# Token mixing of a Fourier layer: seven block products in place of eight, with the running results kept in DRAM

## The chip, the cores and the metric

The kernel runs on one core of one Trainium2 chip. The metric is device time in microseconds (us) of one execution; lower is better. The times below are medians of several executions, and the profile is one further execution with its own time.

## The reference, cut to what matters

There are B = 4 sequences of S = 4224 tokens with D = 192 channels. Three layers follow each other: a token-dependent convolution of 7 taps with softmax weights, a Fourier layer with a small network behind it, and a layer that mixes tokens with two dense matrices. The change is about the last one.

```python
def _moe2_ref(x, w_theta, w_tok_r, w_tok_i, w_ch):
    theta = x @ w_theta
    zr, zi = x * np.cos(theta), x * np.sin(theta)
    yr = np.einsum('ts,bsd->btd', w_tok_r, zr)     # w_tok_r, w_tok_i: 4224 x 4224
    yi = np.einsum('ts,bsd->btd', w_tok_i, zi)
    u = x + yr + yi
    return (u + np.maximum(u @ w_ch, 0.0)).astype(np.float32)
```

So every output token is a sum over 4224 tokens of zr and 4224 tokens of zi, for 4 x 192 = 768 columns.

## The kernel before, in words

The work runs in stages, one after the other: A (convolution and first half of the transform, 11 x 2 steps), B (second half, through DRAM), C (the small network, theta, cos and sin; 33 steps, one for each tile of 128 tokens, which leaves zr and zi in DRAM as `z_scr`), and then the token mix, which takes the last two thirds of the time.

**Token mix.** The 33 input tiles are taken in NG = 11 chunks of three. For one chunk, zr and zi of three input tiles are in SBUF (six blocks of 128 x 768, KQ = 6), and all 33 output tiles n are run through. For each output tile the weights of the six blocks are loaded (`wraw`, 384 KB, in DRAM as `w_mix`). All products are made of two parts to keep precision: a value is split into a rounded high part and the rest. ACT makes the high part of the weights (`wh`, line 935), DVE the low part (`wl = wraw - wh`, line 629), and TensorE does three products for each block (wh zh, wh zl, wl zh, line 1145). With two column halves (batches 0 and 1, batches 2 and 3: a PSUM bank takes 384 columns of them) this makes 6 x 3 x 2 = 36 matmuls for an output tile and chunk, each of a 128 x 128 stationary block of weights and 384 moving columns. DVE then adds the banks to the running result `R`, which lies in SBUF for all 33 tiles (`R[:, n] += banks`, line 634). Three sets of weight buffers and three pairs of banks are used in turn. The blocks zh and zl of the next chunk are made by ACT (line 928) and POOL (line 801) meanwhile.

In the last chunk the result goes into `u3` instead, and the last product with w_ch (transposes and 192-column matmuls) is done between the halves of a tile's 36 matmuls.

The engines run their own programs and meet at semaphores: `w_done` counts finished output tiles, `raw_free` the split weights, `acc_free` the emptied banks, `zraw_free` the split blocks of z. SP issues the loads. Each engine takes its instructions in the order written.

## Time and profile before

| | us |
|---|---|
| median of 3 runs | 3511.55 |
| lowest, highest | 3507.94, 3515.17 |
| the profiled execution, its own time | 3515.86 |
| its span, first to last instruction | 3513.9 |

In the profile PE is TensorE's matmuls, PEld its weight loads, DVE the VectorE, ACT the ScalarE, POOL the GpSimd, SP the engine that issues most DMAs. A window's row says how long each engine was busy in that stretch and with how many instructions. In a timeline row an instruction's start and duration are given; what stands in brackets is how long its engine was idle before it, and what released it. A matmul's duration overlaps with the next one's, so the pace of matmuls is read from their starts or their number, not from their durations.

### The profile page before, as it was taken

Reading aid. Unit: us, or ns where it says so; the run is one execution under the profiler, and the core shown is the slowest. Engines: PE = TensorE matmul, PEld = TensorE weight load, DVE = VectorE, ACT = ScalarE, POOL = GpSimd, SP = SyncE. Lnnn points to the kernel's source line nnn. Section 1 sums busy time; section 2 is a strip of 40 time slices with the busy share of each in tenths; the row PEclk is TensorE's granted clock in tenths of the full one; section 3 lists DMA queues with packets and bytes.
Section 4 is the critical chain, followed back from the end, with each engine's and each line's share of the span. In section 5 each row is a group of like instructions: output and inputs, shape, how many; then the busy total and the mean of one; then the engine's idle time right before and its main releaser. Section 6 shows DMA issues by size and latency. Waiting matters only on the chain.

```text
span 3513.9 us, 51873 instructions
## 1 busy us (share of the span) xinstructions
PE 3249.4 (92%) x18802; PEld 3100.5 (88%) x18802; DVE 1689.8 (48%) x2455; ACT 870.0 (25%) x1319; POOL 737.8 (21%) x718
## 2 busy tenths in 40 slices
PE   3555769999999999999999999999999999999999
PEld 3444338888888999999999999999999999999999
DVE  8998458999997322222222222222222222223444
ACT  1222325555555111111111111111111111112222
POOL 6766015666663110000001000000100000010000
PEclk8777989999999999999999999999999999999999
DMA  5443641111112221222222222222222222222222
GB/s 173 155 170 129 209 164 47 67 58 63 67 66 91 81 85 63 81 72 72 82 69 82 68 81 72 72 81 67 81 67 81 72 73 83 65 84 74 81 90 63
DMA packets 127615, 307.19 MB, mean 87 GB/s; under 512 B 11840, under 2 KB 46720, under 8 KB 127584
## 3 DMA queue, kind: packets, MB, share of 16 engines
q1 hardware_dynamic: 118432, 293.83, 25.7%
q10 hardware_dynamic: 9152, 12.98, 1.3%
q8 instruction: 16, 0.26, 0.0%
q14 instruction: 15, 0.12, 0.0%
HBM read 241.88 MB, written 64.88 MB: 87 GB/s over the span
## 4 chain that ended last, share of the span: by engine, by line
PE 76%; issue 6%; POOLq 5%; DVE 5%; DVEq 3%; DMA 2%; ACT 1%; POOL 1%; ACTq 0%; SPq 0%
PE banks L1145 64%; PE banks L1012 7%; POOLq L744 5%; DVEq L566 2%; DMA fraw<-f_low 2%; DVE angle L613 2%; PE banks L1073 1%; DVE un L622 1%; DVEq L612 1%; POOL head L742 1%; PE banks L1087 1%; DVE angle L610 1%; DVE x2s L567 0%; PE banks L1059 0%; ACT uh L906 0%
## 5 line engine op out<-in xcount | busy, mean ns | idle before, releaser
L1145 PE MATMUL banks<-zh,wh 128*128 128x384 f32 x4356 | 1108.7, 335 | 3.7 <-DVE zl L643 3.4
L1145 PE MATMUL banks<-zl,wh 128*128 128x384 f32 x4356 | 1106.5, 334 | 0.0
L1145 PE MATMUL banks<-zh,wl 128*128 128x384 f32 x4356 | 1106.2, 334 | 0.0
L634 DVE TENSOR_TENSOR R<-R,banks 128x768 f32 (+1 forms) x330 | 314.8, 954 | 1439.7 <-PE banks L1145 1439.7
L1145 PEld LDWEIGHTS banks<-zh,wh 128*128 128x128 f32 x4356 | 783.5, 188 | 5.5 <-DVE zl L643 4.8
L1145 PEld LDWEIGHTS banks<-zl,wh 128*128 128x128 f32 x4356 | 787.6, 188 | 0.0
L1145 PEld LDWEIGHTS banks<-zh,wl 128*128 128x128 f32 x4356 | 787.5, 188 | 0.0
L935 ACT ACTIVATE wh<-wraw 128x768 fp32r<-128x768 f32 x363 | 307.9, 849 | 1709.9 <-PE banks L1145 1709.9
L801 POOL TENSOR_TENSOR zl<-zraw,zh 128x768 f32 x60 | 111.5, 1858 | 1906.4 <-ACT zh L928 1906.4
L629 DVE TENSOR_TENSOR wl<-wraw,wh 128x768 fp32r<-128x768 f32 x363 | 348.3, 960 | 4.2 <-ACT wh L935 4.2
L742 POOL TENSOR_TENSOR head<-head,tap 128x1152 f32<-128x1152 f32 x88 | 231.6, 2631 | 113.7 <-DVE tap L486 100.8
L1023 PE MATMUL banks<-fs,x1s 128*128 128x128 f32 x396 | 90.0, 421 | 178.9 <-DVE x1s L522 178.9
L1023 PEld LDWEIGHTS banks<-fs,x1s 128*128 128x128 f32 x396 | 84.5, 326 | 185.0 <-DVE x1s L522 159.5
L486 DVE TENSOR_TENSOR tap<-xin,banks 128x1152 f32<-128x1152 f32 x132 | 175.6, 1345 | 0.2
L1087 PE MATMUL banks<-w2s,hh 128*128 128x384 f32 x792 | 162.9, 340 | 1.0 <-DVE hl L571 1.0
L889 ACT ACTIVATE hh<-banks 128x512 fp32r<-128x512 f32 x198 | 117.9, 595 | 141.6 <-PE banks L1012 141.6
L571 DVE SCALAR_TENSOR_TENSOR hl<-banks,hh 128x512 fp32r<-128x512 f32 x198 | 135.8, 686 | 25.3 <-ACT hh L889 25.3
L1087 PEld LDWEIGHTS banks<-w2s,hh 128*128 128x128 f32 x792 | 132.8, 189 | 1.2 <-DVE hl L571 1.2
L622 DVE TENSOR_SCALAR un<-R,mv,rstd 128x192 f32 (+1 forms) x132 | 115.5, 934 | 6.1 <-POOL rstd L785 6.1
L686 DVE TENSOR_TENSOR el<-banks,eh 128x256 fp32r<-128x256 f32 x66 | 28.0, 424 | 170.4 <-ACT eh L975 170.4
L1089 PE MATMUL banks<-w2s,hl 128*128 128x192 f32 x792 | 106.9, 270 | 0.0
L1089 PEld LDWEIGHTS banks<-w2s,hl 128*128 128x128 f32 x792 | 106.6, 190 | 0.0
(130 smaller groups left out, 3352.0 us busy)
## 6 DMA issues: line engine op xcount, KB each, us to landing
wraw<-w_mix SPq DMA_DIRECT2D x363, 384.0 KB, 3.0
xin<-x_pad SPq DMA_DIRECT2D x22, 1728.0 KB, 8.1
z_scr<-zsc SPq DMA_DIRECT2D x33, 768.0 KB, 3.4
zraw<-z_scr SPq DMA_DIRECT2D x66, 384.0 KB, 3.7
t_scr<-tst ACTq DMA_DIRECT2D x44, 288.0 KB, 6.0
traw<-t_scr SPq DMA_DIRECT2D x32, 396.0 KB
m_scr<-mst SPq DMA_DIRECT2D x64, 198.0 KB
mbuf<-m_scr SPq DMA_DIRECT2D x33, 384.0 KB, 3.1
```

The source lines that it names most:

```text
L486: return dve.tensor_tensor(four(dst), tap_x(h, k), tap_w(h, k), ALU.mult)
L622: last = dve.tensor_scalar(un[:, b, 0:D], tiles(R, n + 2)[:, b, :], mv[:, b, 0:1], rstd[:, b:b + 1], ALU.subtract, ALU.mult)
L629: dve.tensor_tensor(wl[k][:], wraw[k][:], f32(wh[k][:]), ALU.subtract).then_inc(raw_free, 1)
L634: dve.tensor_tensor(halves(R, n), halves(R, n), banks[:, 2 * k:2 * k + 2, 0:2 * D], ALU.add).then_inc(acc_free, 1)
L742: last = pool.tensor_tensor(head[h][:], head[h][:], tap[k - 1][:], ALU.add)
L744: pool.drain()
L935: act.activation(wh[k][:], wraw[k][:], ACT.Copy).then_inc(wh_ready, 1)
L1012: last = pe.matmul(dst, l, r, start=(t == 0), stop=(t == len(products) - 1))
L1023: last = pe.matmul(bank[i][:, P * j:P * j + P], x1s[h][:, j, P * i:P * i + P], fs[:], start=True, stop=True)
L1087: pe.matmul(bank[4 + b][:, 0:2 * D], hh[:, k, P * b:P * b + P], w2s[:, k], start=(k == 0), stop=False)
L1089: last = pe.matmul(bank[4 + b][:, 0:D], hl[:, k, P * b:P * b + P], w2s[:, k, 0], start=False, stop=(k == HB - 1))
L1145: last = pe.matmul(bank[2 * k + i][:, 0:2 * D], l[k][:, q, :], r[par][:, q, 2 * D * i:2 * D * i + 2 * D], start=(q == 0 and t == 0), stop= ...
```

## The change

The six blocks of a chunk and two neighbouring output tiles (rows 1 and 2) are seen as a 2 x 2 block product. W has blocks W11, W12 (output tile 1: real and imaginary weights) and W21, W22 (output tile 2); Z has Z11, Z12 (zr for the first and second half of the batches) and Z21, Z22 (zi for the same). Instead of eight products of blocks (each three input tiles deep and 384 columns wide) there are seven, of sums of blocks of W and of Z (the form of Strassen and Winograd, which adds up partial sums). A pair of output tiles takes 7 x 3 x 3 = 63 matmuls in place of 72; 16 pairs and the 33rd tile, which is done in the plain way with 36 matmuls, make one chunk.

- A step i of the pair p is called unit i below. Unit i's product goes into a PSUM chain for the pair or into one of two side banks, and products are added to what the bank holds: the running sum in the bank is added to the result after units 0, 2, 4 and 6.
- Each unit's product needs the split of its left operand: ACT `high_w` and DVE `low_w`, 128 x 384 each; four of the seven left operands are sums that POOL makes first (`sum_w`, four adds of 128 x 384). After each unit DVE adds the bank to the result (`add_r`).
- Four of the seven right operands are sums too (`sum_z` on POOL, for one input tile of the next chunk: in the pairs with i4 = 0 of the first three groups of four pairs). All seven are split by ACT (`high_z`) and DVE (`low_z`), in the units that ZPLACE names, in the pairs i4 = 1, 2, 3.
- The results no longer lie in SBUF but in DRAM (`y_scr`). For each pair they are loaded (768 KB) and stored (768 KB). The weights of a pair are 768 KB, as two tiles' were.
- Stage A stores its result to DRAM (`x1_scr`) instead of copying it to `R` with ACT; stage C loads it, adds to it, and stores its own result to `y_scr`. Its loop body holds eight steps instead of one. In its last three steps the z blocks of the first chunk are made already.
- Loads of stage B's and stage C's constants are issued at the start of stage A.
- In the last chunk the w_ch products are laid between the units.

The diff, cut to its core (the parts of stages A to C are left out but for the order of SP's and the last steps):

```diff
-    w_mix = np.stack([blocks(moe2_w_tok_r), blocks(moe2_w_tok_i)], axis=4).reshape(NG * NT, P, KQ * P)
+    br, bi = blocks(moe2_w_tok_r), blocks(moe2_w_tok_i)
+    both = np.stack([br, bi], axis=2)
+    w_pairs = both[:, :2 * NPAIR].reshape(NG, NPAIR, 2, 2, P, 3, P).transpose(0, 1, 4, 2, 3, 5, 6)
...
+        def chain(p):
+            return banks[:, 2 + p % 2, 0:BH]
+        side = (banks[:, 4, 0:BH], banks[:, 5, 0:BH])
+        def dst(p, i):
+            return side[0] if i in (1, 5) else side[1] if i == 3 else chain(p)
+        ADDS = ((0, 0), (1, 1), (0, 1), (0, 0), (1, 1), (0, 1), (1, 0))
+        RAW_OF = {0: 0, 3: 1, 6: 3}
+        SUM_OF = {1: 0, 2: 1, 4: 2, 5: 3}
+        ZPLACE = {1: {1: 0, 3: 1, 5: 2}, 2: {2: 3, 5: 4}, 3: {2: 5, 5: 6}}
...
         @block.sync
+            def step_m(c, jj, i4):
+                p = pair(jj, i4)
+                last = isinstance(jj, int) and jj == 3
+                sp.wait_ge(wl_ready, unit(c, p, 6))
+                load_pair(i4 % 2, NPAIR * c + p + 2)
+                if last and not i4:
+                    load_left(c)
+                if not last and not i4:
+                    sp.wait_ge(zlo_ready, STEPS * (3 * (c + 1) + jj))
+                    load_z(3 * (c + 1) + jj)
+                sp.wait_ge(r_done, mixed(c, p, 6) + 2)
+                sp.dma_start(y_scr[ds(2 * p, 2)].rearrange("i p x -> p i x"),
+                             rbuf[i4][:].rearrange("p i b d -> p i (b d)")).then_inc(r_out[i4], 16)
+                sp.wait_ge(r_out[(i4 + 3) % 4], 16 * (4 * c + jj + 1))
+                load_r((i4 + 3) % 4, p + 3 if not last else (p + 3) % NPAIR)
...
         @block.vector
-            def split_w(c, g, k):
-                dve.wait_ge(wh_ready, NT * c + 3 * g + k + 1)
-                dve.tensor_tensor(wl[k][:], wraw[k][:], f32(wh[k][:]), ALU.subtract).then_inc(raw_free, 1)
-            def add_y(c, n, k):
-                dve.wait_ge(w_done, NT * c + n + 4)
-                dve.tensor_tensor(halves(R, n), halves(R, n), banks[:, 2 * k:2 * k + 2, 0:2 * D],
-                                  ALU.add).then_inc(acc_free, 1)
+            def low_w(c, p, i, k):
+                dve.wait_ge(wh_ready, unit(c, p, i))
+                dve.tensor_tensor(wl[i][:], weights_of(k, i), f32(wh[i][:]), ALU.subtract).then_inc(wl_ready, 1)
+            def low_z(t, par, jj, number):
+                dve.wait_ge(zhi_ready, STEPS * t + (number + 1))
+                o = ZORDER[number]
+                dve.tensor_tensor(z_at(zl, par, o, jj), z_of(o), f32(z_at(zh, par, o, jj)),
+                                  ALU.subtract).then_inc(zlo_ready, 1)
+            def add_r(c, p, k, i):
+                if i == 3:
+                    dve.drain()
+                dve.wait_ge(mm_done, mixed(c, p, i))
+                j, h = ADDS[i]
+                part = half(rbuf[k][:, j], h)
+                dve.tensor_tensor(part, part, dst(k, i), ALU.add).then_inc(r_done, 1)
+            def step_m(c, jj, i4, par):
+                p = pair(jj, i4)
...
+                r_here(c, jj, i4)
+                for i in range(STEPS):
+                    add_r(c, p, i4, i)
...
+                        low_w(c, p + 1, i, (i4 + 1) % 2)
+                    if not last and i in ZPLACE.get(i4, ()):
+                        low_z(3 * (c + 1) + jj, par, jj, ZPLACE[i4][i])
...
         @block.gpsimd
-            def low_z(count, slot, par, q):
-                pool.wait_ge(zh_ready, count)
-                pool.tensor_tensor(zl[par][:, ds(q, 1), :].rearrange("p o x -> p (o x)"), zraw[slot][:],
...
+            def sum_z(t):
+                pool.wait_ge(z_in, 16 * (t + 1))
+                wait(pool, zlo_ready, STEPS * t)
+                zr0, zr1, zi0, zi1 = (zraw[:, q, BH * h:BH * h + BH] for q in range(2) for h in range(2))
+                pool.tensor_tensor(tbuf[:, 0, :], zr1, zr0, ALU.subtract).then_inc(z_sum, 1)
+                pool.drain()
+                pool.tensor_tensor(tbuf[:, 1, :], zi1, tbuf[:, 0, :], ALU.subtract).then_inc(z_sum, 1)
+                pool.tensor_tensor(tbuf[:, 2, :], zi1, zr1, ALU.subtract).then_inc(z_sum, 1)
+                pool.drain()
+                pool.tensor_tensor(tbuf[:, 3, :], zi0, tbuf[:, 1, :], ALU.subtract).then_inc(z_sum, 1)
+            def sum_w(k):
+                w11, w12, w21, w22 = (wraw[k][:, a] for a in range(4))
+                pool.tensor_tensor(wsum[0][:], w21, w22, ALU.add).then_inc(s_sum, 1)
+                pool.drain()
+                pool.tensor_tensor(wsum[1][:], wsum[0][:], w11, ALU.subtract).then_inc(s_sum, 1)
+                pool.tensor_tensor(wsum[2][:], w11, w21, ALU.subtract).then_inc(s_sum, 1)
+                pool.drain()
+                pool.tensor_tensor(wsum[3][:], w12, wsum[1][:], ALU.subtract).then_inc(s_sum, 1)
+            def sums(c, jj, i4):
+                pool.wait_ge(w_in[(i4 + 1) % 2], 16 * (8 * c + 2 * jj + ((i4 + 1) // 2 + 1)))
+                pool.wait_ge(wl_ready, unit(c, pair(jj, i4), 6))
+                sum_w((i4 + 1) % 2)
+            def chunk(c, first=0):
+                with pool.Fori(first, 3) as jj:
+                    for i4 in range(4):
+                        sums(c, jj, i4)
+                        if not i4:
+                            sum_z(3 * (c + 1) + jj)
+                for i4 in range(4):
+                    sums(c, 3, i4)
...
         @block.scalar
+            def high_w(c, p, k, number, i):
+                if i in RAW_OF:
+                    act.wait_ge(w_in[k], 16 * (number + 1))
+                else:
+                    act.wait_ge(s_sum, 4 * (NPAIR * c + p) + (SUM_OF[i] + 1))
+                act.activation(wh[i][:], weights_of(k, i), ACT.Copy).then_inc(wh_ready, 1)
+            def next_w(c, jj, i4, i):
+                act.wait_ge(mm_done, mixed(c, pair(jj, i4), i))
+                high_w(c, pair(jj, i4) + 1, (i4 + 1) % 2, 8 * c + 2 * jj + (i4 + 1) // 2, i)
...
         @block.tensor
-            def mix(c, n, k, par, qs):
-                for q in qs:
-                    for t, (l, r) in enumerate(((wh, zh), (wh, zl), (wl, zh))):
-                        for i in range(2):
...
+            def products(w, dst, par, operand, starts):
+                for q in range(3):
+                    for t, (l, r) in enumerate(((wh, zh), (wh, zl), (wl, zh))):
+                        last = pe.matmul(dst, l[w][:, q, :], r[par][:, operand, q, :], start=starts and q == 0 and t == 0,
+                                         stop=q == 2 and t == 2, skip_group_check=True)
+            def product(c, jj, i4, i, par):
+                p = pair(jj, i4)
+                pe.wait_ge(wl_ready, unit(c, p, i))
+                if i == 1:
+                    pe.wait_ge(r_done, mixed(c, p, -2) + 2)
+                if i == 2:
+                    pe.wait_ge(r_done, mixed(c, p, 0) + 2)
+                if i == 3:
+                    pe.wait_ge(r_done, mixed(c, p, -1) + 2)
+                if i == 4:
+                    pe.wait_ge(r_done, mixed(c, p, 2) + 2)
+                if i == 6:
+                    pe.wait_ge(r_done, mixed(c, p, 4) + 2)
+                products(i, dst(i4, i), par, i, i in (0, 1, 3)).then_inc(mm_done, 1)
```

## Rows read from the trace of the kernel before

**Rows 1.** The page: PE's busy time and instructions; granted clock in 40 slices.

```profile
PE 3249.4 (92%) x18802; PEld 3100.5 (88%) x18802; DVE 1689.8 (48%) x2455; ACT 870.0 (25%) x1319; POOL 737.8 (21%) x718
...
PEclk8777989999999999999999999999999999999999
```

**Rows 2.** Windows: stage B, C, the passage to the mix, mix, last chunk.

```profile
core 0: us, PE busy (x) PEld busy (x) DVE busy (x) ACT busy (x) POOL busy (x), PEclk, DMA share, GB/s
339.00:505.00 166.00, 108.34 (x323) 46.40 (x322) 80.86 (x157) 42.23 (x78) 19.70 (x22) 0.87 0.59 195
520.00:1100.00 580.00, 561.29 (x3563) 507.79 (x3564) 521.57 (x982) 313.51 (x525) 355.59 (x518) 1.00 0.17 59
1100.00:1160.00 60.00, 53.75 (x299) 50.17 (x297) 35.70 (x44) 28.66 (x40) 19.09 (x14) 0.91 0.37 125
1200.00:1700.00 500.00, 500.00 (x2886) 500.00 (x2885) 145.86 (x161) 79.65 (x96) 28.90 (x16) 1.00 0.24 76
3200.00:3490.00 290.00, 290.00 (x1982) 287.88 (x1981) 127.91 (x245) 76.47 (x186) 0.00 (x0) 1.00 0.26 79
```

**Rows 3.** The chain that ended last: start, length, what.

```profile
1160.33 2043.87 PE banks L1145 x11790
```

**Rows 4.** Groups of instructions: line, engine, out<-in, shape, count | busy, mean ns | idle before.

```profile
L1145 PE MATMUL banks<-zh,wh 128*128 128x384 f32 x4356 | 1108.7, 335 | 3.7 <-DVE zl L643 3.4 <-DVE wl L629 0.4
...
L629 DVE TENSOR_TENSOR wl<-wraw,wh 128x768 fp32r<-128x768 f32 x363 | 348.3, 960 | 4.2 <-ACT wh L935 4.2
L634 DVE TENSOR_TENSOR R<-R,banks 128x768 f32 x297 | 283.4, 954 | 1312.9 <-PE banks L1145 1312.9
L742 POOL TENSOR_TENSOR head<-head,tap 128x1152 f32<-128x1152 f32 x88 | 231.6, 2631 | 113.7 <-DVE tap L486 100.8 <-issue 12.0
...
L770 POOL TENSOR_TENSOR zsc<-R,zsc 128x768 f32<-128x768 f32 x33 | 60.9, 1845 | 70.5 <-ACT zsc L921 70.5
```

**Rows 5.** Timeline of PE in stage C: neighbours of five matmuls into one bank.

```profile
1067.69 0.39 PE L1012 MATMUL banks<-ul,w1h 128*128 128x512 f32 x1
1067.92 0.39 PE L1012 MATMUL banks<-uh,w1l 128*128 128x512 f32 x1
```

**Rows 6.** Timeline in the mix: where one output tile ends and the next begins.

```profile
1503.63 0.51 PE L1145 MATMUL banks<-zh,wh 128*128 128x384 f32 x2
1503.83 0.85 ACT L935 ACTIVATE wh<-wraw 128x768 fp32r<-128x768 f32 x1 [5.39 <-PE banks L1145]
1503.93 0.96 DVE L634 TENSOR_TENSOR R<-R,banks 128x768 f32 x1 [4.41 <-PE banks L1145]
...
1504.81 0.95 DVE L629 TENSOR_TENSOR wl<-wraw,wh 128x768 fp32r<-128x768 f32 x1
```

**Rows 7.** Timeline where stage C's end and the mix overlap: POOL and DVE.

```profile
1144.48 1.84 POOL L770 TENSOR_TENSOR zsc<-R,zsc 128x768 f32<-128x768 f32 x1 [20.63 <-ACT zsc L921]
1145.10 2.03 DVE L629 TENSOR_TENSOR wl<-wraw,wh 128x768 fp32r<-128x768 f32 x1 [2.53 <-ACT wh L935]
1146.28 2.56 POOL L771 TENSOR_TENSOR zsc<-R,zsc 128x768 f32<-128x768 f32 x1
```

**Rows 8.** Line 565 in stage C: shortest, median, longest duration in ns.

```profile
L565 DVE TENSOR_TENSOR x2s<-R,banks x66: 540/546/556, 524.1 to 1119.8; 128x384 f32<-128x384 f32 x66
```

**Rows 9.** DMA issues: count, size of one, median us to landing.

```profile
wraw<-w_mix SPq DMA_DIRECT2D x363, 384.0 KB, 3.0
...
z_scr<-zsc SPq DMA_DIRECT2D x33, 768.0 KB, 3.4
```

**Rows 10.** Windows of 1 us in stage A (columns as in rows 2).

```profile
203.00:204.00 1.00, 0.34 (x3) 0.05 (x1) 0.91 (x2) 0.54 (x1) 1.00 (x1) 1.00 0.00 0
...
206.00:207.00 1.00, 0.00 (x0) 0.00 (x0) 0.52 (x1) 0.00 (x0) 1.00 (x1) 0.89 1.01 213
...
209.00:210.00 1.00, 0.00 (x0) 0.00 (x0) 1.00 (x2) 0.00 (x0) 0.00 (x0) 0.50 1.05 414
```

**Rows 11.** The mix's matmuls: durations, first and last start.

```profile
L1145 PE MATMUL banks<-zh,wl x4356: 334/334/522, 1128.3 to 3497.6; 128*128 128x384 f32 x198
```

More of the change, by code:

```diff
@@ new lines, in _, with low_e @@
+            reduce_angle(NT + 1)
+            for i in range(4, STEPS):
+                add_r(0, 0, 0, i)
+                low_w(0, 1, i, 1)
+            for i4 in range(1, 4):
+                step_m(0, 0, i4, 1)
+            dve.wait_ge(rl_in, 16)
+            chunk(0, 0, 1)
+            with dve.Fori(0, (NG - 3) // 2) as c2:
+                chunk(2 * c2 + 1, 1)
+                chunk(2 * c2 + 2, 0)
+            chunk(NG - 2, 1)
+            LAST = NG - 1
+            def low_e(number, u):
+                dve.wait_ge(eh_ready, number)
+                dve.tensor_tensor(el[u % 2][:], banks[:, u % 2, :], f32(eh[u % 2][:]), ALU.subtract).then_inc(el_ready, 1)
@@ L815, in _ @@
+            sums(0, 0, 0)
+            step_c(NT + 2, NT + 2)
+            sum_z(3)
+            for i4 in range(1, 4):
+                sums(0, 0, i4)
+            chunk(0, 1)
+            with pool.Fori(1, NG - 1) as c:
+                chunk(c)
+            with pool.Fori(0, 3) as jj:
+                for i4 in range(4):
+                    sums(NG - 1, jj, i4)
+            for i4 in range(3):
+                sums(NG - 1, 3, i4)
         @block.scalar
@@ new lines, in left_m, with chunk @@
+            def left_m(c):
+                for i in (5, 6):
+                    act.wait_ge(mm_done, mixed(c, NPAIR, i - 4))
+                    high_w(c, NPAIR, 0, 8 * c + 8, i)
+            def chunk(c, par, first=0):
+                with act.Fori(first, 3) as jj:
+                    for i4 in range(4):
+                        step_m(c, jj, i4, 1 - par)
+                for i4 in range(4):
+                    step_m(c, 3, i4, 1 - par)
+                left_m(c)
+            act.sem_inc(wh_ready, 2)
@@ new lines, in _, with high_e @@
+            for i4 in range(1, 4):
+                step_m(0, 0, i4, 1)
+            chunk(0, 0, 1)
+            with act.Fori(0, (NG - 3) // 2) as c2:
+                chunk(2 * c2 + 1, 1)
+                chunk(2 * c2 + 2, 0)
+            chunk(NG - 2, 1)
+            LAST = NG - 1
+            def high_e(number, u):
+                act.wait_ge(et_ready, number)
+                wait(act, ep_ready, number - 2)
+                act.activation(eh[u % 2][:], banks[:, u % 2, :], ACT.Copy).then_inc(eh_ready, 1)
@@ L1006, in _ @@
+            high_pair(NPAIR, 1)
         @block.tensor
@@ new lines, in left_m, with chunk @@
+            def left_m(c, par):
+                for i in range(3):
+                    left(c, i, par)
+            def chunk(c, par, first=0):
+                with pe.Fori(first, 3) as jj:
+                    for i4 in range(4):
+                        step_m(c, jj, i4, par)
+                for i4 in range(4):
+                    step_m(c, 3, i4, par)
+                left_m(c, par)
+            run_c(step_c, pe)
+            pe.wait_ge(zlo_ready, 3 * STEPS)
+            product(0, 0, 0, 0, 0)
@@ new lines, in _ @@
+            transpose_x2(NT, 0)
+            product(0, 0, 0, 1, 0)
+            transpose_x2(NT, 1)
+            product(0, 0, 0, 2, 0)
+            theta_product(NT)
+            for i in range(3, STEPS):
+                product(0, 0, 0, i, 0)
+            for i4 in range(1, 4):
+                step_m(0, 0, i4, 0)
+            chunk(0, 0, 1)
+            with pe.Fori(0, (NG - 3) // 2) as c2:
+                chunk(2 * c2 + 1, 1)
+                chunk(2 * c2 + 2, 0)
+            chunk(NG - 2, 1)
```

1010 lines of the change are left out of this document (580 added, 430 removed).

## The prediction, written before the changed kernel had run

> **What bounds the kernel now.** I read the page first, then windows by stage, then the chain. The page gives PE 92% of the span; DVE has 48% [rows 1]. That is a mean over stages, so the windows decide. In the mix PE is busy 500.00 of 500 us with 2886 matmuls, DVE 146, ACT 80, POOL 29, at full granted clock; the last chunk has PE at 290 of 290 [rows 2]. The reader should see that nothing but PE counts there: the chain runs through 11790 matmuls in 2043.87 us without a break [rows 3]. The pace is 500/2886 = 0.1733 us a matmul. Stage C has PE at 561 of 580 but DVE at 522 and POOL at 356 as well: three full engines [rows 2].
>
> **What is removed.** Before: 11 chunks x 33 tiles x 36 = 13068 matmuls (three groups of 4356, one of them in [rows 4]). After: 11 x (16 x 63 + 36) = 11484, of the same 128 x 384 form. 1584 fewer at 0.1733 us is 274.5 us. Nine in a row now go into one bank where two banks alternated. The nearest rows are two of five 512-column matmuls into one bank: starts 0.23 us apart [rows 5], 0.449 ns a column, against 0.1733/384 = 0.451. So no price for that, and none for smaller groups as long as what PE waits for is there.
>
> **What PE now waits for.** A unit is 9 matmuls, 1.56 us; a pair is 7 units, 10.92. Product i of a pair adds into a bank that DVE must have read after unit i-2, so an add has one unit of time. Where a tile ends, ACT starts 0.20 and DVE 0.30 us after the next matmul's start [rows 6]. A DVE add of 384 columns with one source in PSUM takes 0.546 [rows 8]; low_w with 384, both sources in SBUF, I take as line 629's 0.951 less the 0.408 by which 768 and 384 columns differ on PSUM (0.954 of line 634 less 0.546) = 0.54. DVE starts its next one 0.07 before the recorded end (0.88 apart for 0.96) [rows 6], so 0.47 of time each. A unit asks 0.94 us of DVE in 1.56; the add is done at 0.85 of 1.56. Alone this is hidden: bound below nothing.
>
> **POOL and DVE.** Before, POOL had 28.9 of 500 us [rows 2]. Now it has four sums of 384 columns a pair. From 1152 columns at 2.631 and 768 at 1.845 [rows 4] a 384-column one is 1.06, or 1.02 from start to start (1146.28 less 1144.48 is 1.80 for a recorded 1.84). Line 629, whose mean is 0.960 [rows 4], once took 2.03 while POOL's add ran [rows 7]: it ended 0.95 after POOL's, and POOL's next add then took 2.56 instead of 1.84. So one waits for the whole of the other, and the waiting one goes next. Line 565, with one source in PSUM, ran beside POOL for all of stage C and never took over 0.556 [rows 8]. So add_r is free of this, low_w and low_z are not. The Trainium skill, in "SBUF — State Buffer", section "Who interferes with whom", has it as a rule: a DVE instruction with two SBUF inputs and a GpSimd one that reads SBUF exclude each other for the whole instruction, with at most one SBUF input they don't. Were there no such exclusion, the stop worked out below would be 0.9 us instead of 3.4, and the sum 3264 with the clock's full; by the rule it is the sum below, and the trace agrees with the rule. In an ordinary pair the waits are short: POOL's adds fit into the gaps between low_w's, each low_w waits 0.1 to 0.3 us, the add still comes before 1.56. Free.
>
> **The place where it is not free: sum_z.** POOL takes things in order, and after the weight sums of a pair i4 = 0 it stands at sum_z's wait for z. When does z land? At the start of pair i4 = 0 SP issues, in this order: the store of a pair's results, the load of another's, a pair's weights, then z: 4 x 0.786 = 3.15 MB on one queue, from 1.0 us on. A saturated microsecond moved 0.414 MB [rows 10], so 7.6 us; the part before the first data is 1.4 to 2.1 (3.0 for 0.39 MB, 3.4 for 0.79 MB [rows 9]). z lands at 1.0 + 1.7 + 7.6 = 10.3, 0.6 before the pair ends. From the start of pair i4 = 1 (0.0) on:
> - four sums of z: 4 x 1.02, two drains (no row; I take 0.15 each, 0 to 0.3), and DVE's low_w between them, about 1.2 in all: done at 5.0. Then the first weight sum: 6.0.
> - In unit 1 ACT waits for that sum, copies (0.1 + 0.47, half of line 935's 0.85 and a little [rows 6]), DVE's low_w waits behind it, and queued behind low_w in DVE's program are low_z and the add of unit 2. low_w: 0.13 + 0.45 for POOL's second sum + 0.47; POOL's third sum goes next, 1.02; low_z 0.47; the add 0.55 + 0.05. Total 6.0 + 3.7 = 9.7.
> - PE may start product 4 at 4 x 1.56 = 6.24. It waits 3.4 us.
> This comes three times in each of the first ten chunks, 30 times: 102 us. Without DVE's turns it is 0.9 us; with z 2 us later it is 5 or more.
>
> **The clock.** A stretch without matmuls costs more than itself if the clock falls. In stage A PE stopped in 203 to 204, and the clock was still 0.89 in 206 to 207 and 0.50 in 209 to 210 [rows 10]. That is the lower level, 1.2 GHz, reached after more than 3 us; 3.4 us is on the edge. In the passage to the mix 6.25 us without PE went with a clock of 0.91 over 60 us, 10.8 us at half speed, up to 5.4 us lost [rows 2]: 0.86 us for each idle one. Bounds for a stop are so 0 and 2.9 us; I take 0.8, as single stops of this length are nearest to stage A's row, where it only just fell: 24 us.
>
> **The rest.** In stage C x1's load and y's store lie in the DMA's 0.17 share [rows 2]. Its DVE has 90%, so the seven low_z of steps 30 to 32 cost up to 3.3 us each by DVE's time; steps 31 and 32 have no normalising left to do, so some 3 us in all. The passage to the mix loses about 6.5 us now (13068 x 0.1733 = 2264.7 and the last chunk's 3.12 a tile, some 100, against 1126.9 to 3497.8 [rows 11]); afterwards that is shorter, but pair 2's weights are issued only after the last z store, and I expect the same loss. ACT's copies to R in stage A stood on no path. The tail may be 3 us shorter. Together 0, from -12 to +15.
>
> **Sum.** The profiled execution: 3515.9 - 274.5 + 102 + 24 + 0 = 3367. The median of the runs lies 4.3 below the profiled one: **3363 us**.
>
> **Rivals.**
> 1. *POOL's lateness is mostly hidden* (z lands before POOL has finished the weight sums, or a 384-column sum is nearer 0.9): stops under 1.5 us, clock full. 3237 + 30 x 0 to 1.5 = 3237 to 3282. For it: transfers of 0.786 MB landed in 3.4 us when alone. Against: four stand in one queue.
> 2. *The stops are long* (z 2 us later, or the clock falls at nearly each one): 6.3 us or more a time, 3237 + 190 and over: 3430 to 3500.
> 3. *Code loading at loop ends.* PE's loop body grows from 108 matmuls to 252, with as many weight loads. If each of 21 backward jumps cost a DMA's landing, by the shortest rows here 3.0 us less PE's run-ahead, that is 0 to 63 us, so up to 3426; with the stops at my value, 3400. Against: the last chunk's body, already larger than the others, loses nothing (290 of 290 [rows 2]). The Trainium skill, "Runtime: NRT & Kernel Launch", section "Instruction fetch mechanics", says that a taken branch to code outside the fetched window forces a fetch; no row here shows such a stop.
> 4. *DMA becomes the bound*, the other side. A chunk moves 16 x 2.36 + 3 x 0.79 + 0.39 = 40.5 MB. It took 33 x 36 x 0.1733 = 205.9 us; under 197 GB/s it takes longer. Stage B sustained only 195 [rows 2]: then 207.7 a chunk, 3512 + 20 = 3532. Against: stage B had a share of 0.59, and 414 GB/s has been moved [rows 10].
>
> POOL's and DVE's exclusion alone can't make it slower: all of POOL's 76 sums in a chunk added to DVE's 245 operations, 77.5 + 115.2 = 192.7 us, is still below 205.9.
>
> **Chances.** Forecast (3282 to 3430) 0.57; rival 1 0.20; rival 2 0.10; rival 3 0.06; rival 4 0.04; the rest, a time within 0.2% (7 us, about what a measurement of this kernel can tell from no change), 0.03. The forecast's own range is 3300 to 3430. The 8 in 10 range takes in the upper part of rival 1, and rival 3: 3262 to 3440. Faster 0.93, same 0.03, slower 0.04.
>
> **What would show it.** Right: 11484 matmuls of the mix; PE near 97% in a mix window, not 100; stops of some 3 us before product 4, about 44 us apart with a gap at the end of each chunk, released by DVE's add; DVE just before idle behind ACT's high_w, ACT behind POOL's sum, POOL behind z's DMA; low_w's with more than 1 us; the last chunk, without sum_z, with no stops. Wrong: a busy share of 100% (rival 1), a clock well below 1.00 in the mix (rival 2), stops at loop ends released by nothing (rival 3), a DMA share near 1 (rival 4). It would also be wrong if the add after a unit came late in ordinary pairs: 0.2 us in each of the 176 would be 35 us more.

## The result, and the profile after

The changed kernel takes 3410.06 us (median of 4 runs, 3408.26 to 3414.97), against 3513.16 for the kernel before on the same chip: a ratio of 0.9711, 95% interval 0.9694 to 0.9728. It is faster, by 103 us; 3363 was predicted, with a range of 3262 to 3440.

The page of the kernel after, to be put beside [rows 1]: busy time of the engines, and the granted clock in 40 slices.

```profile
PE 3026.9 (89%) x17218; PEld 2867.3 (84%) x17218; DVE 2680.5 (79%) x4407; ACT 1244.2 (36%) x2320; POOL 1538.7 (45%) x1494
...
PEclk8777889999999899999999999999999999999999
```

PE has 1584 instructions fewer and is busy 222 us less, DVE is busy 991 us more. The windows answer to [rows 2]: stage C, the passage, two stretches of the mix and the last chunk.

```profile
core 0: us, PE busy (x) PEld busy (x) DVE busy (x) ACT busy (x) POOL busy (x), PEclk, DMA share, GB/s
520.00:1100.00 580.00, 556.26 (x3507) 501.84 (x3506) 522.03 (x982) 314.50 (x528) 359.22 (x525) 1.00 0.30 104
1100.00:1160.00 60.00, 42.66 (x255) 38.54 (x253) 46.16 (x60) 28.78 (x52) 30.19 (x23) 0.92 0.32 112
1200.00:1700.00 500.00, 483.17 (x2711) 480.54 (x2711) 397.90 (x656) 179.96 (x356) 217.59 (x200) 0.97 0.58 210
1700.00:2200.00 500.00, 470.43 (x2631) 466.80 (x2630) 376.20 (x626) 170.67 (x336) 205.34 (x189) 0.97 0.57 203
3130.00:3390.00 260.00, 260.00 (x1796) 258.89 (x1795) 185.19 (x332) 105.35 (x228) 61.42 (x57) 1.00 0.37 125
```

The mix no longer has PE at 500 of 500. It does 2711 and 2631 matmuls where 2886 had been done, and the clock is at 0.97. The last chunk, which prepares no further z, is full. So the loss lies in the chunks that prepare z for the next one, and at the passage. Who releases PE in 1200 to 3120, and whom POOL waits for (total, times, longest):

```profile
PE banks L1452 <- DVE rbuf L785: 58.5, 29, 3.2
PE banks L1452 <- issue: 23.1, 6, 4.7
...
POOL tbuf L982 <- DMA zraw<-z_scr: 122.5, 29, 5.8
```

Twenty of the 29 stops for DVE's add are of 2.4 to 3.2 us, the nine at the first quarter of a chunk of 1.25 or less: there the 36 matmuls of the left tile lie between the transfers. One of the twenty, in the timeline (start, length, engine, what; idle before and what ended it):

```profile
1287.46 1.02 POOL L982 TENSOR_TENSOR tbuf<-zraw 128x384 f32<-128x384 f32 x1 [4.82 <-DMA zraw<-z_scr]
...
1292.00 1.01 POOL L992 TENSOR_TENSOR wsum<-wraw 128x384 f32<-128x384 f32 x1
...
1293.04 0.53 ACT L1160 ACTIVATE wh<-wsum 128x384 fp32r<-128x384 f32 x1 [3.22 <-POOL wsum L992]
...
1293.60 0.99 DVE L723 TENSOR_TENSOR wl<-wsum,wh 128x384 fp32r<-128x384 f32 x1 [1.97 <-ACT wh L1160]
1294.52 1.35 DVE L728 TENSOR_TENSOR zl<-zraw,zh 128x384 f32 x1
1295.79 0.54 DVE L785 TENSOR_TENSOR rbuf<-rbuf,banks 128x384 f32<-128x384 f32 x1
...
1296.47 0.47 PE L1452 MATMUL banks<-zh,wh 128*128 128x384 f32 x1 [2.62 <-DVE rbuf L785]
```

This is read from the end. PE waits for an add; the add stands in DVE's program behind a split of z and a split of a weight sum; that one waits for ACT's copy, the copy for POOL's sum, and POOL had stood 4.82 us for z. Note the two splits: 0.99 and 1.35 us for operations that take 0.55 elsewhere. What the clock did around it (PE's busy time and instructions, granted clock, DMA share, GB/s), and where the slow stretch ends:

```profile
1294.00:1297.00 3.00, 0.53 (x2) 0.95 0.59 243
1297.00:1300.00 3.00, 3.00 (x11) 0.50 0.00 0
1300.00:1304.00 4.00, 4.00 (x24) 0.99 0.00 0
...
1300.19 0.34 PE L1452 MATMUL banks<-zh,wh 128*128 128x384 f32 x1
```

After the stop some 3 us at 0.50, which is the 1.2 GHz level: 11 matmuls where the full clock does 17. From start to start, 1296.47 to 1300.19, twelve matmuls take 3.72 us where 12 x 0.1733 is 2.08: 1.6 us more on top of the stop. The clock fell so at 18 of the twenty stops.

The six stops that end in "issue" lie at PE's outer loop over two chunks, two for each of its three backward jumps. The first pair of them, and what the two DMA queues that carry instructions moved during the first one (packets, MB, share):

```profile
1760.65 0.48 PE L1452 MATMUL banks<-zh,wh 128*128 128x384 f32 x1 [4.68 <-issue]
1765.64 0.48 PE L1452 MATMUL banks<-zl,wh 128*128 128x384 f32 x1 [3.55 <-issue]
...
q8 instruction: 2, 0.03, 4.8%
q14 instruction: 3, 0.02, 2.6%
```

Three more instruction packets move in the second stop. From 1417 to 1523, where PE jumps back twice in its inner loop, these queues move nothing.

The passage to the mix: first PE's two long stops, then POOL, ACT and SP.

```profile
1164.47 0.66 PE L1452 MATMUL banks<-zh,wh 128*128 128x384 f32 x1 [10.84 <-DVE rbuf L785]
1199.34 0.66 PE L1452 MATMUL banks<-zh,wh 128*128 128x384 f32 x1 [17.36 <-DVE rbuf L785]
...
1155.55 1.80 POOL L1006 TENSOR_TENSOR zsc<-UR,zsc 128x768 f32<-128x768 f32 x1 [15.04 <-ACT zsc L1152]
1161.30 0.99 POOL L992 TENSOR_TENSOR wsum<-wraw 128x384 f32<-128x384 f32 x1
...
1190.68 0.99 POOL L982 TENSOR_TENSOR tbuf<-zraw 128x384 f32<-128x384 f32 x1 [14.05 <-DMA zraw<-z_scr]
...
1187.36 0.52 ACT L1160 ACTIVATE wh<-wraw 128x384 fp32r<-128x384 f32 x1 [13.49 <-DMA wraw<-w_pairs]
1195.97 0.52 ACT L1160 ACTIVATE wh<-wsum 128x384 fp32r<-128x384 f32 x1 [8.10 <-POOL wsum L992]
...
1159.45 17.57 SPq L491 DMA_DIRECT2D z_scr<-zsc  x2
1181.19 0.37 SPq L464 DMA_DIRECT2D wraw<-w_pairs  x1
```

POOL has the weight sums of pair 1 behind its z products, for which it waited 15.04 us; that ends in the stop of 10.84. Pair 2's weights are asked for at 1181.19, behind the last store of z, and z of the fourth tile 0.7 us later. Both are late, but the stop of 17.36 hangs on z: ACT has the raw weights at 1187.36, while POOL stands at z until 1190.68, then makes its sums, and only then the weight sum that ACT copies at 1195.97. Last, two groups of DVE (busy, mean ns, idle before) and two transfers (size, median us from issue to landing):

```profile
L723 DVE TENSOR_TENSOR wl<-wsum,wh 128x384 fp32r<-128x384 f32 x664 | 522.3, 787 | 96.8 <-ACT wh L1160 71.3
L723 DVE TENSOR_TENSOR wl<-wraw,wh 128x384 fp32r<-128x384 f32 x498 | 302.8, 608 | 29.5 <-ACT wh L1160 21.1
...
z_scr<-zsc SPq DMA_DIRECT2D x33, 768.0 KB, 3.4
zraw<-z_scr SPq DMA_DIRECT2D x33, 768.0 KB, 7.4
```

### The profile page after: what moved, and what is told of

Its sections match the earlier page's. It is cut to its first block, busy times and chain, and to the rows that moved or that the text cites. A ratio compares the mean times of both kernels' runs of the same rounds, so it can differ in the third digit from the quotient of the medians.

```text
span 3412.8 us, 57572 instructions
## 1 busy us (share of the span) xinstructions
PE 3026.9 (89%) x17218; PEld 2867.3 (84%) x17218; DVE 2680.5 (79%) x4407; ACT 1244.2 (36%) x2320; POOL 1538.7 (45%) x1494
## 4 chain that ended last, share of the span: by engine, by line
PE 60%; DVE 9%; issue 8%; POOLq 8%; DMA 6%; DVEq 3%; ACT 2%; POOL 2%; SPq 2%; ACTq 1%
PE banks L1452 48%; PE banks L1319 7%; POOLq L960 5%; DMA zraw<-z_scr 4%; DVE un L773 3%; DVE zl L728 2%; DVE angle L716 1%; PE banks L1380 1%; DMA fraw<-f_low 1%; POOLq L993 1%; DVEq L698 1%; DVEq L715 1%; POOL head L958 1%; PE banks L1533 1%; PE banks L1394 1%
## 5 line engine op out<-in xcount | busy, mean ns | idle before, releaser
L1452 PE MATMUL banks<-zh,wh 128*128 128x384 f32 x3828 | 1310.1, 342 | 107.6 <-DVE rbuf L785 91.4
L1452 PE MATMUL banks<-zl,wh 128*128 128x384 f32 x3828 | 1298.4, 339 | 10.9 <-issue 10.9
L1452 PE MATMUL banks<-zh,wl 128*128 128x384 f32 x3828 | 1299.0, 339 | 0.0
L785 DVE TENSOR_TENSOR rbuf<-rbuf,banks 128x384 f32<-128x384 f32 x1168 | 644.1, 551 | 309.0 <-PE banks L1452 281.9
L1160 ACT ACTIVATE wh<-wsum 128x384 fp32r<-128x384 f32 x704 | 370.2, 526 | 883.5 <-PE banks L1452 758.9
L992 POOL TENSOR_TENSOR wsum<-wraw 128x384 f32<-128x384 f32 x176 | 179.4, 1019 | 1096.5 <-DVE wl L723 971.0
L723 DVE TENSOR_TENSOR wl<-wsum,wh 128x384 fp32r<-128x384 f32 x664 | 522.3, 787 | 96.8 <-ACT wh L1160 71.3
L1160 ACT ACTIVATE wh<-wraw 128x384 fp32r<-128x384 f32 x528 | 278.0, 526 | 490.3 <-PE banks L1452 476.8
L723 DVE TENSOR_TENSOR wl<-wraw,wh 128x384 fp32r<-128x384 f32 x498 | 302.8, 608 | 29.5 <-ACT wh L1160 21.1
L994 POOL TENSOR_TENSOR wsum<-wsum,wraw 128x384 f32<-128x384 f32 x176 | 212.1, 1205 | 28.0 <-issue 28.0
L997 POOL TENSOR_TENSOR wsum<-wraw,wsum 128x384 f32<-128x384 f32 x176 | 199.0, 1131 | 28.0 <-issue 28.0
L995 POOL TENSOR_TENSOR wsum<-wraw 128x384 f32<-128x384 f32 x176 | 186.9, 1062 | 0.0
```

Source lines behind the costliest of these rows:

```text
L723: dve.tensor_tensor(wl[i][:], weights_of(k, i), f32(wh[i][:]), ALU.subtract).then_inc(wl_ready, 1)
L785: dve.tensor_tensor(part, part, dst(k, i), ALU.add).then_inc(r_done, 1)
L992: pool.tensor_tensor(wsum[0][:], w21, w22, ALU.add).then_inc(s_sum, 1)
L994: pool.tensor_tensor(wsum[1][:], wsum[0][:], w11, ALU.subtract).then_inc(s_sum, 1)
L995: pool.tensor_tensor(wsum[2][:], w11, w21, ALU.subtract).then_inc(s_sum, 1)
L997: pool.tensor_tensor(wsum[3][:], w12, wsum[1][:], ALU.subtract).then_inc(s_sum, 1)
```

## The experiments

Times are medians of the runs; "before" took 3514 to 3516 us in each series. Unless it says otherwise an edit is made to the changed kernel (3410 us).

**The late z, by moving its sums.** GpSimd takes the weight sums of the next pair first.

```diff
                     for i4 in range(4):
                         sums(c, jj, i4)
-                        if not i4:
+                        if i4 == 1:
                             sum_z(3 * (c + 1) + jj)
...
```

The part left out does the same for the first chunk.

> GpSimd forms the sums of z one pair later: behind the weight sums asked for at the second pair of the four (i4 = 1) in place of the first. In the profile after, TensorE stops 29 times for VectorE's add at L785 (58.5 us in all), where GpSimd stood 29 times at the z sums for the z load (122.5 us) with the next pair's weight sums queued behind it. Theory A (the late z load is the cause): these 29 stops go, and with them most of the some 40 us that the clock lost behind them: 3315 us, between 3300 and 3335. Theory B (GpSimd's sums slow VectorE's splits of the weights, and that makes the stops): the same sums run, so little moves: 3385 to 3415 us.

Measured: 3352.62 us, ratio to before 0.9542 (0.9526 to 0.9558), 57 us less. PE's waits in 1200 to 3300:

```profile
PE banks L1453 <- DVE rbuf L785: 31.7, 58, 0.7
```

The 29 stops of up to 3.2 us are gone and the clock of 1240 to 1700 is 1.00, but 58 of 0.5 to 0.7 us stand in their place. The time lies between both theories: the late z is a cause and not all of it. The same edit turned the 17.36 us stop of the passage into one of 10.35, with the weights' load where it was: z was that stop's last link.

**The late z, by moving its load.**

```diff
                 sp.wait_ge(wl_ready, unit(c, p, 6))
-                load_pair(i4 % 2, NPAIR * c + p + 2)
-                if last and not i4:
-                    load_left(c)
                 if not last and not i4:
                     sp.wait_ge(zlo_ready, STEPS * (3 * (c + 1) + jj))
                     load_z(3 * (c + 1) + jj)
+                load_pair(i4 % 2, NPAIR * c + p + 2)
+                if last and not i4:
+                    load_left(c)
```

> SyncE asks for z ahead of the next pair's weights (768 KB) in place of behind them. Theory A (the late z load is the cause of the 29 stops): z was asked for 0.7 us later and landed behind the weights; it now lands some 2 us earlier, so stops of 2.4 to 3.2 us shrink to 0.4 to 1.2 us: 3355 us, between 3335 and 3380, and the idle time of TensorE for L785 falls from 58.5 to some 15 to 25 us. Theory C (the load of z is slow because of the stores and loads of the running results around it, not because of the weights ahead of it): z lands 0.7 us earlier at most: 3390 to 3405 us.

Measured: 3353.83 us, ratio 0.9547 (0.9531 to 0.9563); 29 stops, 31.0 us in all, the longest 1.3, where 15 to 25 us had been expected. Theory A holds and C falls. But POOL still waits for z, half as long as before (122.5 us in the kernel of the change):

```profile
POOL tbuf L982 <- DMA zraw<-z_scr: 61.2, 23, 3.3
```

So the twenty large stops fall from 2.6 to 1.25 us, and what is left of them is still in part the late load. This and the run before it end within 1.3 us of each other.

**GpSimd without reads.** Each sum becomes three fills. In the weight sums (those of z alike):

```diff
-                w11, w12, w21, w22 = (wraw[k][:, a] for a in range(4))
-                pool.tensor_tensor(wsum[0][:], w21, w22, ALU.add).then_inc(s_sum, 1)
...
+                for a in range(4):
+                    for again in range(3):
+                        pool.drain()
+                        last = pool.memset(wsum[a][:], 0.25)
+                    last.then_inc(s_sum, 1)
```

> The kernel of the change, but this one leaves out GpSimd's sums of weights and of z in the mix: in the place of each stand three fills of the same tile with a constant (and one difference over 8 columns at the head of each group), so GpSimd writes for about as long but hardly reads. Theory B (GpSimd's two-input operations slow VectorE's two-input operations that lie in SBUF alone): the split of a weight sum, 0.79 us on the average in the mix, falls to 0.55 to 0.60 us. Theory A (the late z load makes the 29 stops): GpSimd still stands at z for the load, so most of the 29 stops stay, each shorter by the 0.2 to 0.7 us that the splits gain; the two theories are not exclusive, and the run says how the 2.0 us of a mean stop divides. If B is wrong, the mean stays at 0.75 us or above.

DVE's two groups, and who releases PE:

```profile
L723 DVE TENSOR_TENSOR wl<-wsum,wh 128x384 fp32r<-128x384 f32 x575 | 320.9, 558 | 194.5 <-ACT wh L1165 153.1
L723 DVE TENSOR_TENSOR wl<-wraw,wh 128x384 fp32r<-128x384 f32 x432 | 240.6, 557 | 12.7 <-ACT wh L1165 4.2
...
PE banks L1457 <- DVE rbuf L785: 109.8, 26, 5.7
```

In the same stretch the kernel of the change has 0.796 us for the first group. It falls to 0.558, as theory B has it, and every group of splits now has a mean of 0.556 to 0.559. But the stand-in was not as long as the sums: 0.42 us a fill with drains between makes some 1.4 us a sum in place of 1.1, so POOL ends later and the stops are longer, 3472.03 us in its one run. The division of a stop between load and access can't be read here; the run with the same line alone, below, does it.

**PE's outer loop written out.**

```diff
-            with pe.Fori(0, (NG - 3) // 2) as c2:
+            for c2 in range((NG - 3) // 2):
                 chunk(2 * c2 + 1, 1)
                 chunk(2 * c2 + 2, 0)
```

> TensorE's outer loop over two chunks a turn is written out, so that TensorE jumps back there no more; its inner loops over the three quarters of a chunk stay, as do the loops of all other engines. Theory (each of the three backward jumps costs TensorE two stops for nothing that the profile shows, 23.1 us in all, and some 27 us at half clock, worth about 14): 3373 us, between 3365 and 3385. Rival (these stops come with each first pass of code, not with the jump): the written out code stops at as many or more places: 3400 us or more.

Measured: 3384.18 us, ratio 0.9633 (0.9616 to 0.9649). No stop of PE is released by "issue" any more: the jump is the cause. 26 us are won and not 37, since 31 stops for DVE's add now take 70.2 us instead of 58.5 for 29. Three of them (1.94, 2.03 and 2.48 us) are new and lie where PE's own jumps were. There DVE stands in its turn for nothing that the profile shows, 3.3 to 3.8 us:

```profile
1752.75 0.55 DVE L785 TENSOR_TENSOR rbuf<-rbuf,banks 128x384 f32<-128x384 f32 x1 [3.29 <-issue]
```

DVE's outer loop over two chunks jumps back at these places; in the kernel of the change DVE waits for PE there.

**The passage, GpSimd's side, then both sides.** To the first edit the second adds SyncE's, for which SyncE's first chunk is written out (left out here).

```diff
             step_c(NT, NT)
-            step_c(NT + 1, NT + 1)
             sums(0, 0, 0)
+            step_c(NT + 1, NT + 1)
             step_c(NT + 2, NT + 2)
```

```diff
-            for n in range(NT, NT + 3):
+            step_c(NT, NT)
+            sp.wait_ge(wl_ready, unit(0, 0, 6))
+            load_pair(0, 2)
+            for n in range(NT + 1, NT + 3):
                 step_c(n, n)
...
```

> GpSimd alone: the weight sums for pair 1 stand one step earlier in its order, ahead of the second last step of the stage before. In the profile after, ScalarE waited 8.1 us for them and TensorE stopped for 10.84 us at 1164.47. Theory: that stop goes, with most of the 13.7 us at half clock behind it: 12 to 16 us less, 3396 us (3390 to 3401). Rival: the 17.36 us stop at 1199.34 is for pair 2's weights, which SyncE issues late; it hangs on SyncE alone, TensorE only gets there sooner and waits longer: 0 to 4 us less.

(The wait of 8.1 us is misread here: it is the one at 1195.97, for pair 2's weight sum. For pair 1's ACT waited 6.57 us.)

> The edit of the run before, and SyncE loads pair 2's weights ahead of its last two steps of the stage before, in place of behind the waits for the last stores of that stage. Theory: both stops at the passage go (10.84 and 17.36 us) with most of the 34 us at half clock behind them: 30 to 40 us less, 3375 us (3367 to 3383). Rival: a store of y or z then waits behind SyncE's wait for the weights' buffer, and the stop comes back there: less than 15 us gained.

Measured: 3404.83 us (0.9691, 0.9671 to 0.9712) and 3401.31 us (0.9690, 0.9667 to 0.9713). Their intervals overlap with that of the kernel of the change: 5 and 9 us are hardly told from nothing, and the 12 to 16 and the 30 to 40 are missed. The 10.84 us stop fell to 6.83 in both. The trace of the second says why no more came.

```profile
1168.09 0.97 SPq L472 DMA_DIRECT2D zraw<-z_scr  x1
...
1180.96 0.52 ACT L1171 ACTIVATE wh<-wsum 128x384 fp32r<-128x384 f32 x1 [18.89 <-POOL wsum L1003]
...
1184.32 0.66 PE L1463 MATMUL banks<-zh,wh 128*128 128x384 f32 x1 [14.85 <-DVE rbuf L796]
```

The weights of pair 2 are there, but z of the fourth tile is still asked for behind the last store of z, POOL stands at it, and the 17.36 us stop returns as one of 14.85. It was a third thing late behind the same store, 0.7 us behind the weights, which I had not looked for, though the profile after shows it. Less than 15 us were gained, as the rival had it, but not by its mechanism: no store stood behind SyncE's wait for the buffer; the load of z had not been moved.

**All three edits.**

> Together: z sums one pair later, both edits of the passage, TensorE's outer loop written out. Theory: the gains add, as they lie in different places: 95 + 35 + 37 us less, 3245 us (3230 to 3270). Rival: with the stops gone VectorE (79% busy in the mix) is the next limit and gives back part: 3270 to 3310 us.

Measured: 3325.74 us, ratio 0.9457 (0.9442 to 0.9472). The gains measured one by one were 57.4, 8.8 and 25.9, together 92; 84 came. Both ranges of the expectation are missed; what is left in the mix are the small stops, 61 of 39.6 us in all. All but the three at DVE's loop (2.05, 2.10 and 2.89 us) lie where DVE splits z while POOL forms sums.

**The splits of z moved to where POOL is idle**, on top of the three edits.

```diff
-        ZPLACE = {1: {1: 0, 3: 1, 5: 2}, 2: {2: 3, 5: 4}, 3: {2: 5, 5: 6}}
+        ZPLACE = {1: {6: 0}, 2: {3: 1, 5: 2, 6: 3}, 3: {3: 4, 5: 5, 6: 6}}
```

> The run with all three edits, and the seven splits of z moved to steps of the pair in which GpSimd forms no sums (numbers 0; 1, 2, 3; 4, 5, 6 at the second, third and fourth pair, steps 3 to 6, in place of steps 1 to 5). In the run with all three edits TensorE still stopped 61 times for VectorE's add (39.6 us), at 0.72 and 0.49 us twice per load of z, where the splits of a weight sum took 1.25 us and that of z 1.37 us beside GpSimd's sums, in place of 0.55. Theory B (the shared access is all that is left): these stops go: 3292 us (3284 to 3300). Rival (VectorE is simply full in those pairs): the stops move with the splits: 3318 us or more.

Measured: 3270.82 us, ratio 0.9299 (0.9285 to 0.9313), 55 us less from a line that changes no work at all, and 13 less than the theory's range. The split of raw z, in the run before it and in this one:

```profile
L739 DVE TENSOR_TENSOR zl<-zraw,zh 128x384 f32 x87 | 95.1, 1094 | 0.0
```

```profile
L739 DVE TENSOR_TENSOR zl<-zraw,zh 128x384 f32 x87 | 48.4, 556 | 0.0
```

1.094 us becomes 0.556, and in 1200 to 3100 only 3 stops are left, 6.7 us. That is 33 us of stops. A stop costs more than its idle time: in the run with three edits, matmuls around one of 0.72 us start at 1271.14 and 1272.20: 1.06, less 0.17 of pace, is 0.89 lost. The next starts at 1272.45, another 0.08 late. That is 0.25 more for each of 58 stops, 15 us. Another 4 us came from a shorter passage (the table below).

The splits of weight sums are still at 0.786 us on the average beside POOL's sums, and cost PE nothing there. The three stops that are left lie at DVE's outer loop, one at each backward jump. The first:

```profile
1707.63 0.56 DVE L796 TENSOR_TENSOR rbuf<-rbuf,banks 128x384 f32<-128x384 f32 x1 [3.34 <-issue]
```

Instruction packets move there as well (4 from 1704 to 1708). No run writes that loop out, so what it would give is open.

**The same line alone.**

> The kernel of the change with the later places of the splits of z as its one edit; z is still loaded late and GpSimd's sums of it still stand ahead of the weight sums. In a stop of the kernel after, VectorE's split of z took 1.35 us between the late split of the weights and the add that TensorE waits for. Theory (load wait and shared access add up in one chain, and both must be paid): the 29 stops stay and are 1.2 us shorter, so they are near 1.3 us and the clock, as in the run with z loaded first (stops of 1.07 us), no longer falls behind them: 3345 us (3330 to 3365). Rival (the stops are the load's alone): TensorE waits as long, 3395 us or more. Rival (the splits were all of it, since they hold VectorE back before z has landed): no stops, 3320 us or less.

Measured: 3349.10 us, ratio 0.9523 (0.9507 to 0.9539). Leaving out one stop of the passage (16.55 us), PE waits 20 times for DVE's add from 1200 on, 28.3 us in all: fifteen of 1.2 to 1.4 us, five of 1.7 to 2.5. POOL still waits 118.3 us for z. The nine small stops are gone, which the theory had kept. Both rivals fall. A large stop of 2.6 us is thus a sum: take z's split out of the chain and 1.3 stays; halve the wait for z and 1.25 stays; take the weight sums out from behind z's load, and stops of 0.4 to 0.7 stay, which go when z's splits move too (the run before). Behind the stops of 1.3 us the clock did not fall in either run, so each edit alone gives 56 to 61 us.

**Two more edits at the passage**, on top of the four. "The run before this" in the expectation is the one with four edits (3270.82 us), whose time was not known when it was written.

```diff
             load_pair(0, 2)
+            sp.wait_ge(zlo_ready, 3 * STEPS)
+            load_z(3)
...
             keep_x2(NT)
+            next_w(0, 0, 0, 0)
+            next_w(0, 0, 0, 1)
             keep_theta(NT)
             sines(NT)
-            for i in range(4):
+            for i in range(2, 4):
                 next_w(0, 0, 0, i)
```

> The run before this, and two edits at the passage into the mix. SyncE loads the z of the fourth tile ahead of the last stores of the stage before (it was issued at 1169.9, behind the last store of z, landed at 1177.8, and TensorE stopped 9.42 us for it). ScalarE splits the first two weights of the second pair ahead of the last but one sines (VectorE stood 4.29 us for the first, TensorE 6.83 us). Theory: 9 and 4 us, and a part of the clock behind them: 3278 us (3272 to 3286), 14 us under the run before it. Rival: another link of the passage (GpSimd's z products, VectorE's angles) holds TensorE as long: 3290 us or more.

Measured: 3262.64 us, ratio 0.9281 (0.9268 to 0.9294), 8 us less than the run with four edits, where 14 had been expected. It is the fastest of all, 147 us under the kernel of the change. Its mix is near the limit again:

```profile
1200.00:1700.00 500.00, 498.00 (x2873) 497.57 (x2872) 408.05 (x686) 188.26 (x370) 243.19 (x209) 1.00 0.63 226
2200.00:2700.00 500.00, 497.25 (x2868) 496.77 (x2867) 409.63 (x686) 187.66 (x369) 237.21 (x206) 1.00 0.62 222
```

## Why the prediction was right, and where its terms were off

The time lies in the range and in the forecast's case, and the mechanism forecast is the one that the trace shows. But the 47 us between 3363 and 3410 come from terms that were wrong both ways, so that it came as near as this is in part luck.

For the account I count from the traces what PE lost between its matmuls: the distance between the starts of two neighbours, less 0.1733 us (for other shapes, less their usual distance). What is lost at a stop and by slow matmuls behind it goes to that stop. As a check, 1240 to 3120 of the kernel of the change:

```profile
1240.00:3120.00 1880.00, 1798.41 (x10095) 0.97 0.58 209
```

1880 less 10095 x 0.1733 is 131 us; the count gives 96.5 and 31.4 of them to the two kinds of stop. The passage ends after 340 matmuls of the mix, ahead of the next stop for z. In us, each from one execution:

| kernel | first mix matmul at | passage | DVE's add, chunks 0 to 9 | "issue" at PE's outer loop |
|---|---|---|---|---|
| before | 1126.9 | 8.6 | 0 | 0 |
| the change | 1136.8 | 44.8 | 96.5 | 31.4 |
| z sums later | 1130.2 | 38.3 | 47.0 | 30.3 |
| z loaded first | 1133.6 | 42.3 | 38.7 | 29.4 |
| PE's outer loop written out | 1126.2 | 47.0 | 105.6 | 0 |
| both sides of the passage | 1126.2 | 39.4 | 97.9 | 33.0 |
| three edits | 1127.1 | 34.9 | 57.5 | 0 |
| and z's splits moved | 1126.0 | 30.9 | 11.7 | 0 |
| and two more at the passage | 1124.3 | 23.7 | 10.6 | 0 |
| z's splits moved alone | 1136.3 | 44.8 | 36.8 | 31.6 |

- **What is removed**: 11484 matmuls, as counted, and in the run with all edits 2873 of them in 500 us, 0.174 us each. Nine in a row into one bank cost nothing. Right.
- **The place: sum_z.** Every link of the chain is in the trace: add behind splits, split behind ACT, ACT behind POOL's sum, POOL behind z. Counting back from PE's stop (1293.85 where it began, 6.24 of pair i4 = 1, 10.92 of the pair before), z landed 10.8 us after its pair began; 10.3 was worked out. The stop is 2.6 us, not 3.4. POOL took 4.5 us for the z sums where 5.6 were worked out (from 0.6 before the pair to 5.0 in it), since DVE's turns between them cost about 0.2 and not 1.2; the two gaps that stand for the drains are 0.16 each, as taken. DVE's late split of a weight and its split of z took 2.2 us together, not 2.5. And there are 20 of this size, not 30, since a chunk's first quarter has the left tile's matmuls as cover, which the prediction overlooked. Idle time 58.5 us for the 102 predicted.
- **The clock**: it fell behind 18 of the twenty, for some 3 us each. 0.8 a stop was taken; clock and restart cost 1.6 at the stop shown, and 38 us in all where 24 were taken. Stops and clock together: 96.5 us for 126, 30 less.
- **POOL and DVE** exclude each other as [rows 7] had it, now shown by taking the reads away (0.796 to 0.558 us) and by moving z's splits away from them (1.094 to 0.556). The section "Who interferes with whom" of the Trainium skill's "SBUF — State Buffer" says the same, and these two runs agree with it. But the prediction went on to "Free" for ordinary pairs with z's splits in them and priced the exclusion only inside the long stop. Measured, once the load is out of the way, it makes 58 stops more.
- **The rest, term "passage to the mix, the same loss"**: this is the step that failed. It was taken as 6.5 us and is 45. PE stopped there, after its first mix matmul, for 35.1 us (2.15, 1.97, 10.84, 1.55, 1.23, 17.36). I had seen that pair 2's weights are issued after the last z store, and had not asked what each thing issued behind that store holds up: the weights, z of the fourth tile, and on POOL the sums of pair 1 behind the z products. The clock was at 0.50 for 34 us around the two long stops, but PE stood for two thirds of that, which costs nothing more; the slow matmuls lost 8 us. So the loss is 38 us over the term. The first two edits at this place won 5 of it and the last two 7 (8.8 and 8.2 in the medians, each near the least that can be told); in the fastest run the passage still loses 24.
- **Rival 3, code loading**: it was there beside the forecast and not in place of it, with a chance of 0.06. Its price was right in kind and wrong in place: 19 jumps of the inner loops (252 matmuls a turn) cost nothing, the three of the outer loop (two chunks a turn) 23.1 us of stops, 31 with the slow matmuls; 26 us were won by writing it out, and VectorE's own jumps, three stops of 6.5 us in all, took the place. "Against: the last chunk's body loses nothing" was no evidence, since that body has no such jump. The Trainium skill, "Runtime: NRT & Kernel Launch", "Instruction fetch mechanics", says that a taken branch whose target lies outside the fetched window forces a fetch. The trace agrees at these three jumps, where instruction packets move during the stops, and at the inner loops, where none do from 1417 to 1523. For which engine they move the trace does not say, and how large that window is no run here shows.
- **Rivals 1, 2 and 4** fell. z did not land in 3.4 us but in 7.4 from its issue; no z stop of this kernel passed 3.2 us, though the clock did fall at nearly each one, which was one of rival 2's two conditions; and the DMA was no bound: in the fastest run it moved 226 GB/s at a share of 0.63 with PE at 498 of 500, above the 197 that the prediction gave as the need.
- **Slips of reading** that change nothing above: in [rows 7] line 629 ended 0.81 us after POOL's add (1147.13 less 1146.32), not 0.95; 3.4 less the three turns of DVE and POOL (1.2, 0.45, 1.02) is 0.7 and not 0.9.
- The first mix matmul starts at 1136.8, 9.9 later than before. That is one execution's own: four of the kernels above with the same code up to there start it at 1126.2, 1130.2, 1133.6 and 1136.3.

In the profiled execution, 3415 us for the 3367 predicted, the 48 us are: passage 38, outer loop 31, z and its clock 30 less, the first matmul's place 10, the end behind the last matmul 5 less (10.9 us for 16.3). That is 44; 4 stay without a row.

The late z and the splits beside POOL, taken away one after the other, gave 57 and 55 us, 112 together, while the stops for DVE's add fell only from 96.5 to 11.7, by 85. The table shows the rest. On these stops the two edits won 49.5 and 45.8; between them, with PE's outer loop written out, VectorE's own jumps had added some 10. The passage gave 7 and 4 more, and what is left is the place of the first matmul and what single executions differ by.

## What to carry to other kernels

When a change replaces the bound engine's work by work of its helpers, look for the places where a helper stands in order behind a transfer: follow each queue one place past every wait, at the passage between stages too, and price all that is issued behind the same store. Splits and sums of two engines that exclude each other should lie in different parts of the period; here one line of places was worth 55 us, and the later sums of z 57. What a stop costs beside its idle time depends on its size: the stops of the change, most of them with a fall of the clock behind them, cost 1.65 times their idle time (96.5 us for 58.5), those of 1.3 us and less without it 1.25 times (38.7 for 31.0), and the 58 small ones 1.5 times (47.0 for 31.7). So halving the large stops by either of their two causes took some 60 of the 96.5 us away. Where a loop's jump stops one engine, look at the same loop of the others: here VectorE's came out once TensorE's was gone.

## What the runs showed of the hardware that was not expected

- PE's jump back of a loop with 1,080 matmuls in its code made two stops, at the first jump 4.68 and 3.55 us, 5.0 us apart; jumps over 252 matmuls made none. DVE's jump back of its loop over the same two chunks stopped DVE for 3.3 to 4.0 us.
- Of twenty single stops of 2.4 to 3.2 us, 18 were followed by 3 to 7 us at half clock, and in the run with z's splits moved those of 1.98 and 2.03 us were too. No single stop under 1.9 us in the mix of any kernel in the table was followed by any.
- At half clock the matmuls of 384 columns started 0.32 us apart and not 0.173, so a microsecond at half clock costs less than half of one, and one in which PE stands anyway costs nothing.
- A stop of 0.72 us of PE cost 0.89 from start to start: with the next matmul's later start the restart costs 0.25 us, which adds up over 58 stops.
- Each 768 KB load of z took 7.4 us to land behind three other transfers of that size, while the queue moved mostly 370 to 450 GB/s; the 768 KB stores of z, with fewer neighbours, took 3.4.
